# Attention scores from chunk 5 on as one float32r product a head, over q and k stacked three times

## The reference

```python
# q, k, v: (4, 8, 768, 40); i_gate, f_gate: (4, 8, 768); all float32
for t in range(S):
    m_new = np.maximum(f_gate[:, :, t] + m, i_gate[:, :, t])
    f_stab = np.exp(f_gate[:, :, t] + m - m_new)
    i_stab = np.exp(i_gate[:, :, t] - m_new)
    m = m_new
    C = f_stab[:, :, None, None] * C + i_stab[:, :, None, None] * np.einsum('bhd,bhe->bhde', vt, kt)
    n = f_stab[:, :, None] * n + i_stab[:, :, None] * kt
    h_tilde = np.einsum('bhde,bhe->bhd', C, qt)
    nq = np.einsum('bhd,bhd->bh', n, qt)[:, :, None]
    y[:, :, t] = sigmoid(o_gate[:, :, t]) * h_tilde / np.maximum(np.abs(nq), 1.0)
x = y as (3072 tokens, 320)
h = x @ w_in; g = np.maximum(h, 0) + alpha * np.minimum(h, 0)   # 320 -> 2048
x = g @ w_out                                                  # 2048 -> 320
h = np.maximum(np.maximum(x @ w1, x @ w2), x @ w3)             # 320 -> 768, three times
out = h @ w_out2                                               # 768 -> 320
```

## Time and profile before

| what | value |
|---|---|
| median of 3 runs | 748.95 us |
| profiled execution's own time | 748.46 us |
| its span (first to last instruction) | 746.7 us |
| PE busy | 737.6 us (99%) |
| PE weight loads busy | 652.4 us (87%) |
| DVE busy | 455.0 us (61%) |
| ACT busy | 306.9 us (41%) |
| POOL busy | 175.4 us (23%) |
| moved by DMA | 55.66 MB, mean 75 GB/s |

### The profile page before, as it was taken

One profiled execution on the slowest core, in us unless ns is written; L12 is line 12 of the kernel. 1 busy time (PEld: TensorE's weight loads), 2 busy tenths in 40 slices (PEclk: granted clock), 3 DMA queues, 4 the chain that ended last, 5 costly groups with the idle time before them and its releaser, 6 DMA issues.

```text
span 746.7 us, 11542 instructions
## 1 busy us (share of the span) xinstructions
PE 737.6 (99%) x4430; PEld 652.4 (87%) x4430; DVE 455.0 (61%) x774; ACT 306.9 (41%) x646; POOL 175.4 (23%) x201
## 2 busy tenths in 40 slices
PE   8899999999999999999999999999999999999998
PEld 6899999999988888888888888888888888888886
DVE  7787787799778868776877548633242424324232
ACT  6675744645564446444643446311212112121211
POOL 6697154164243324332431000000000000000000
PEclk9999999999999999999999999999999999999999
DMA  9973322423223213221200270030202002000101
GB/s 237 287 206 110 120 67 66 124 71 98 96 86 105 75 39 119 92 87 35 67 2 0 103 218 0 1 120 2 77 1 77 1 1 78 1 35 1 36 1 35
DMA packets 30407, 55.66 MB, mean 75 GB/s; under 512 B 3176, under 2 KB 19024, under 8 KB 29968
## 3 DMA queue, kind: packets, MB, share of 16 engines
q1 hardware_dynamic: 29888, 54.49, 23.8%
q10 hardware_dynamic: 464, 0.43, 0.2%
HBM read 46.96 MB, written 7.95 MB: 74 GB/s over the span
## 4 chain that ended last, share of the span: by engine, by line
PE 90%; DVE 4%; POOL 2%; issue 2%; ACT 2%; DMA 1%; SPq 0%; DVEq 0%; ACTq 0%; POOLq 0%
PE bank L794 26%; PE bank L757 22%; PE bank L680 6%; PE bank L772 6%; PE bank L774 5%; PE bank L773 5%; PE bank L809 3%; PE bank L810 3%; PE bank L811 3%; PE bank L776 3%; PE bank L777 3%; PE bank L688 2%; PE bank L696 1%; PE bank L718 1%; PE bank L730 1%
## 5 line engine op out<-in xcount | busy, mean ns | idle before, releaser
L757 PE MATMUL bank<-x_split,w_hi 128*128 128x512 f32 (+2 forms) x560 | 167.4, 366 | 2.0 <-ACT x_split L898 2.0
L757 PE MATMUL bank<-x_split,w_lo 128*128 128x512 f32 (+2 forms) x336 | 120.1, 360 | 0.0
L940 ACT ACTIVATE g_full<-bank 128x512 f32<-128x512 f32 (+2 forms) x112 | 59.8, 534 | 135.4 <-PE bank L757 134.4
L757 PEld LDWEIGHTS bank<-x_split,w_hi 128*128 128x128 f32 x560 | 102.6, 189 | 14.5 <-ACT x_split L898 2.2
L1184 DVE SCALAR_TENSOR_TENSOR g_full<-g_full,beta,bank 128x512 f32<-128x512 f32 (+2 forms) x112 | 74.6, 666 | 40.7 <-ACT g_full L940 40.1
L1165 DVE TENSOR_TENSOR g_lo<-g_full,g_hi 128x512 fp32r<-128x512 f32 (+2 forms) x112 | 79.5, 710 | 32.5 <-ACT g_hi L949 31.7
L1205 DVE TENSOR_TENSOR best<-bank,first_of_max 128x512 f32<-128x512 f32 x36 | 24.9, 692 | 102.5 <-PE bank L794 76.1
L772 PE MATMUL bank<-g_hi,wproj 128*128 128x512 f32 (+2 forms) x224 | 83.9, 374 | 0.8 <-DVE g_lo L1165 0.8
L949 ACT ACTIVATE g_hi<-g_full 128x512 fp32r<-128x512 f32 (+2 forms) x112 | 63.1, 564 | 48.1 <-DVE g_full L1184 47.9
L774 PE MATMUL bank<-g_hi,wproj 128*128 128x512 f32 (+2 forms) x224 | 80.5, 359 | 0.0
L773 PE MATMUL bank<-g_lo,wproj 128*128 128x512 f32 (+2 forms) x224 | 80.3, 358 | 0.0
(11 more groups left out here) (135 smaller groups left out, 1379.7 us busy)
## 6 DMA issues: line engine op xcount, KB each, us to landing
u_bcast<-u_scratch SPq DMA_DIRECT2D x21, 512.0 KB, 3.9
kv<-in_kv SPq DMA_DIRECT2D x24, 324.0 KB, 3.0
q_t<-in_q_t SPq DMA_DIRECT2D x24, 180.0 KB
k_t<-in_k_t SPq DMA_DIRECT2D x72, 60.0 KB
out<-final SPq DMA_DIRECT2D x5, 640.0 KB, 3.8
wproj_raw<-in_w_out SPq DMA_DIRECT2D x4, 640.0 KB, 11.1
o_gate<-in_o_gate SPq DMA_DIRECT2D x4, 640.0 KB, 4.5
w_raw<-in_w_max SPq DMA_DIRECT2D x2, 1152.0 KB, 6.4
```

The costliest lines, as they stand in the source:

```text
L757: ins = pe.matmul(ps[:, 0:cols], w[:, a, f], xs[:, x, 0:cols], start=(m == 0), stop=(m == 7))
L940: act.activation(gf[:, n % GF_SLOTS, 0:cols], hid[j % HID_BANKS][:, 0:cols], ACT.Relu, scale=-1.0).then_inc(neg_done, 1)
```

## The change

From chunk 5 (`STACK`) on, q and k come from HBM transposed, 40 rows for all 8 heads side by side, three times below each other (120 x 1024 values, 480 KB each), into one buffer `qk_raw` (it lies where the k slots were, so it is filled after the last plain scores). ACT copies both into float32r tiles `qk_terms`, with a sign by row: q as (high, high, -high), k as (high, -high, high). Then a masked add turns the negative rows into low parts: DVE does q (one scalar_tensor_tensor over 120 x 1024), POOL does k (a product with a row mask, then an add, over 120 x 1024 each). One float32r matmul a head over the 120 rows then gives high x high + high x low + low x high. The per-slot k loads go away for these chunks; q stays, for `carry`.

```diff
 def chunk_groups(ch):
...
-    return [[("scores", ch)] + soon * [("prepare", ch + 1)], [("carry", ch)],
+    stack, begin = STACK < ch + 1 < NCH, ch + 1 == STACK
+    return [[("scores", ch)] + soon * [("prepare", ch + 1)], [("carry", ch)] + stack * [("high", ch + 1)],
             [("values", ch)] + more * [("gate", ch + 1, 0)],
             more * [("gate", ch + 1, 1)] + [("finish", ch, 0)],
-            [("finish", ch, 1)] + pack * [("pack", ch + 1, 0)] + later * [("prepare", ch + 2)],
-            pack * [("pack", ch + 1, 1)]]
+            [("finish", ch, 1)] + begin * [("high", ch + 1)] + stack * [("low", ch + 1)]
+            + pack * [("pack", ch + 1, 0)] + later * [("prepare", ch + 2)],
+            begin * [("low", ch + 1)] + pack * [("pack", ch + 1, 1)]]
...
+        raw, kt_at = sb("qk_raw", [128, 2, H, L], F32)
+        terms3, _ = sb("qk_terms", [128, 2, H, L], F32R)
...
             eng.dma_start(qt[0:KR, c, :, :], q_t[ch]).then_inc(qk_loaded[c], 16)
-            for a in range(KH):
-                eng.dma_start(kt[a * D:(a + 1) * D, c, a * NK:(a + 1) * NK, :], k_t[ch, a]).then_inc(qk_loaded[c], 16)
+            if ch < STACK:
+                for a in range(KH):
+                    eng.dma_start(kt[a * D:(a + 1) * D, c, a * NK:(a + 1) * NK, :], k_t[ch, a]
+                                  ).then_inc(qk_loaded[c], 16)
...
+        def load_raw(eng, ch):
+            eng.wait_ge(scored, NG * STACK)
+            wait(eng, q_terms, ch - STACK)
+            wait(eng, k_terms, ch - STACK)
+            for n in range(2):
+                eng.dma_start(raw[0:KR, n, :, :].rearrange("p h t -> p (h t)"), qk[ch - STACK, n]
+                              ).then_inc(raw_loaded, 16)
...
                 load_chunk(sp, ch)
                 load_u(sp, ch)
+                if ch > STACK:
+                    load_raw(sp, ch - 1)
...
-                    pe.wait_ge(qk_loaded[c], QK_LOADS * nth)
+                    if ch < STACK:
+                        pe.wait_ge(qk_loaded[c], qk_loads(ch))
+                    else:
+                        pe.wait_ge(q_terms, ch - STACK + 1)
+                        pe.wait_ge(k_terms, ch - STACK + 1)
...
+                            if ch < STACK:
+                                lhs, rhs = kt[0:KR, c, h % KH * NK + h // KH, :], qt[0:KR, c, h // KH, :]
+                            else:
+                                lhs, rhs = terms3[0:KR, 1, h, :], terms3[0:KR, 0, h, :]
...
+                if kind == "high":
+                    act.wait_ge(raw_loaded, 32 * (n + 1))
+                    act.wait_ge(scored, NG * ch)
+                    act.activation(terms3[0:KR, 0, :, :], raw[0:KR, 0, :, :], ACT.Copy, scale=sign[0:KR, 1:2]
+                                   ).then_inc(qk_high, 1)
+                    act.activation(terms3[0:KR, 1, :, :], raw[0:KR, 1, :, :], ACT.Copy, scale=sign[0:KR, 0:1]
+                                   ).then_inc(qk_high, 1)
...
+                if kind == "low":
+                    dve.wait_ge(qk_high, 2 * (ch - STACK) + 1)
+                    dve.scalar_tensor_tensor(out=terms3[0:KR, 0, :, :], in0=raw[0:KR, 0, :, :], scalar=own[0:KR, 0, 2:3],
+                                             in1=terms3[0:KR, 0, :, :].bitcast(F32), op0=ALU.mult, op1=ALU.add
+                                             ).then_inc(q_terms, 1)
...
+                if kind == "low":
+                    pool.wait_ge(qk_high, 2 * (ch - STACK) + 2)
+                    link(pool.tensor_scalar(raw[0:KR, 1, :, :], raw[0:KR, 1, :, :], own[0:KR, 0, 1:2], None, ALU.mult))
+                    pool.tensor_tensor(terms3[0:KR, 1, :, :], raw[0:KR, 1, :, :], terms3[0:KR, 1, :, :].bitcast(F32),
+                                       ALU.add).then_inc(k_terms, 1)
```

More of the change, by code:

```diff
@@ L63 @@
 UNSPLIT = FIRST[2]
+STACK = UNSPLIT
+TERMS = 3
 STILL = 18
@@ L67 @@
 RING_BANKS = 3
-QK_LOADS = 16 * (1 + KH)
 CREDIT2 = 2
@@ L183, with qk_loads @@
 W2_LOW_AT = {5: (0,), 6: (1, 2), 7: (3, 4), 8: (5, 6), 9: (7, 8), 10: (9, 10), 11: (11,)}
+def qk_loads(ch):
+    return sum(16 * (1 + KH) if n < STACK else 16 for n in range(ch % SLOTS, ch + 1, SLOTS))
 class Links:
@@ L211, in of_heads, with build @@
     return ps.rearrange("p (g w) -> p g w", g=NK)[:, :, 0:KH * DE].rearrange("p g (k d) -> p g k d", k=KH)
-def build(nc, f_g, i_g, q_t, k_t, kv, o_g, w_in, w_out, alpha, w_max, w_out2, out):
+def build(nc, f_g, i_g, q_t, k_t, qk, kv, o_g, w_in, w_out, alpha, w_max, w_out2, out):
     with ExitStack() as ctx:
@@ L350, in build @@
         qk_loaded = [sem(f"qk_loaded{c}") for c in range(SLOTS)]
+        raw_loaded = sem("raw_loaded")
+        sign_set = sem("sign_set")
+        qk_high = sem("qk_high")
+        q_terms = sem("q_terms")
+        k_terms = sem("k_terms")
         u_loaded = [sem(f"u_loaded{c}") for c in range(SLOTS)]
@@ L535, in _ @@
                             load_o(sp, b + 3)
+            load_raw(sp, NCH - 1)
             sp.wait_ge(x_ready, NCH)
@@ L679, in attention @@
                             h = g * HG + k
-                            ins = pe.matmul(ps[:, k * L:(k + 1) * L], kt[0:KR, c, h % KH * NK + h // KH, :], qt[0:KR, c, h // KH, :],
-                                            start=True, stop=True)
+                            if ch < STACK:
+                                lhs, rhs = kt[0:KR, c, h % KH * NK + h // KH, :], qt[0:KR, c, h // KH, :]
+                            else:
+                                lhs, rhs = terms3[0:KR, 1, h, :], terms3[0:KR, 0, h, :]
+                            ins = pe.matmul(ps[:, k * L:(k + 1) * L], lhs, rhs, start=True, stop=True)
                         ins.then_inc(scored, 1)
@@ L877, in attention @@
                 nth = ch // SLOTS + 1
+                if kind == "high":
+                    n = ch - STACK
+                    if n == 0:
+                        act.wait_ge(sign_set, 1)
+                    act.wait_ge(raw_loaded, 32 * (n + 1))
[4 more added lines that the diff above has]
+                                   ).then_inc(qk_high, 1)
                 if kind == "sigmoid":
@@ L1063, in attention @@
                 kind = step[0]
-                if kind in ("prepare", "gate", "pack", "sigmoid", "exps", "turns", "bcast", "products"):
+                if kind in ("prepare", "high", "gate", "pack", "sigmoid", "exps", "turns", "bcast", "products"):
                     return
@@ L1101, in attention @@
                     dve.wait_ge(alpha_loaded, 16)
+                    dve.tensor_scalar(sign[:, :], own[:, 0, 1:3], -2.0, 1.0, ALU.mult, ALU.add).then_inc(sign_set, 1)
                     link(dve.tensor_scalar(beta[:, :], alpha_sb[:, :], -1.0, 1.0, ALU.mult, ALU.add))
@@ L1387, in nine, with three @@
         return rows.reshape(NCH, NK, KH, D, L)
+    def three(x):
+        rows = chunks(x).transpose(0, 2, 4, 1, 3).reshape(NCH, D, H * L)[STACK:]
+        return np.concatenate([rows] * TERMS, axis=1)
     arrays = {
@@ L1393 @@
         "q_t": nine(q).transpose(0, 2, 3, 1, 4).reshape(NCH, KR, NK, L),
-        "k_t": nine(k).transpose(0, 2, 3, 1, 4),
+        "k_t": nine(k).transpose(0, 2, 3, 1, 4)[:STACK],
+        "qk": np.stack([three(q), three(k)], axis=1),
         "kv": np.concatenate([tokens(k), tokens(np.concatenate([v, np.ones_like(v[..., :1])], axis=3))], axis=2),
```

5 lines of the change are left out of this document (4 added, 1 removed).

## The result

The changed kernel takes **838.98 us** (median, 837.87 to 839.89) against 748.25 for the kernel before, a ratio of 1.121 (95% interval 1.119 to 1.123). The forecast was 757 with a range of 742 to 770: the side was right, the size was not. The loss is 91 us instead of 8.

A forecast was written before the change was run, and what follows sets the result against it. PE, busy 99% of the span, was taken as the bound. The terms -16.2 + 14.6 + 5.2 + 2.1 + 2.5 + 1.6 gave +9.8 us, 758.8 on the median's scale, less 2 for overlap: 757 us, range 742 to 770.

The forecast's parts named there:

- The gain: Scores on PE: 8 float32r records of 106 ns replace 16 float32 ones, 0.85 us a chunk, 19 chunks, -16.2 us.
- both rivals on the width: Scores on PE: narrow float32r as slow as float32, 770 us, chance 0.14; or quicker weight load, 753 us, chance 0.08.
- (a): First chunk change in each block: q's low part comes late behind ACT's gapless run, lengthened by the copies; +14.6 us.
- (d): POOL against DVE: POOL's extra work slows DVE by 0.5 us in five of ten waiting chunks; +2.5 us, 0 to 8.
- (b): Later chunk changes in a block: PE's scores wait for q's low part behind `y`, or for the buffer loop; +5.2 us.
- (b), the loop: One buffer, low part to low part: 15 us; waits of 1.95 and 1.2 us in block 2, hidden in 512-column blocks.
- the loop binds everywhere: Rival: slower loads or locked-out DVE make the buffer loop cost 2 us more at 14 chunks; 775 us, chance 0.06.
- (c): End of block 0: the first copies on ACT have no cover; +2.1 us, 0 to 3.3.
- (e): PE's granted clock: one fall to half speed for 3.3 us after a wait; +1.6 us, 0 to 6.
- The rival on the clock: The clock falls at all five long waits instead of one, 4 x 1.6 us more; 763 us, chance 0.09.
- The far end of the gain: Scores on PE at 0.06 us a head: the gain's far end is -22 us, another 6 us on PE.
- What would show it: Signs in the later profile; forecast wrong if low-part waits sum below 14 us or POOL's low part of k comes last.

The follow-up runs named there:

- compute_q: The changed kernel without the loads after chunk 5's and without POOL's low part of k; copies and q's low part stay: 773.2 us.
- load_once: The changed kernel with q and k loaded once, for chunk 5; copies and low parts still made for every chunk: 800.3 us.
- warm_q: compute_q plus 72 float32r products of 512 columns, sums thrown away, put into PE's six long waits: 764.0 us (ratio 1.019 to 1.022).
- the versions with moves: Against the changed kernel: q and k loaded once in 80 rows, laid into 120 rows by six SBUF moves; 742.6 to 802.5 us by order and first chunk.

## Why the forecast missed

*The gain* (-16.2): 14.9 us in 18 chunks, 15.7 for 19. Right, and with it 0.106 us a record; both rivals on the width are out.

*(a), the first chunk change of a block* (+14.6): 15.7 us without POOL's work (`compute_q`), so the part with ACT's run was right. In the whole change it is 24.6, and the same without the loads (24.7, `load_once`): 9 us come from DVE's waits for POOL, which (a) left to (d).

*(b)*: the waits behind `y` read from the earlier trace rows are right in order and low in sum (7.3 us measured without the loop, 4.8 read). DVE's low part took up to 2.1 us beside POOL and not 1.2, which accounts for part of it.

*(b), the loop* is the step that failed first. The forecast made it 15 us and called it hidden in the blocks of 512 columns. It is 20.2: issue and loads 6.5 instead of 5.0 (the upper end, 6.2, was in the text, and not used), copies 2.2 instead of 2.1, and from the split to the end of the low part 11.6 instead of 8.0. Of these last 3.6 us 1.8 are `g_lo` at 2.40 instead of 0.60, 1.3 the two `norm` at 0.96 and 0.68 instead of 0.17. The rival "the loop binds everywhere" had the mechanism, at a chance of 0.06 and 2 us a chunk; inside a block it exceeds the old distance of the later chunks, 17 us and less, by 3 us and more. The working of that rival is off too: 2 us at 14 chunks are 28, and even less the 5.2 of (b) that makes 780, not 775.

*(c)* (+2.1): the copies cost 1.2 us there (`compute_q`, 82.02 against 80.80); the other 4.5 us of 5.7 came with POOL's work, as a stop of PE and a lower clock behind it.

*(d), POOL against DVE* (+2.5) failed as well, by two sizes. POOL needs 5.3 us a chunk, not 3.5 to 4.6, and a meeting costs up to 1.9 us (`g_lo`, `inner`), not 0.5; and it was counted in waiting chunks only, where it also lengthens the loop. The loads and POOL's work together are 65.8 us (`compute_q` to the whole change) against 3 forecast, 2.5 for POOL and 0.5 for the loop: 23.1 are waits for q's low part, 16.8 waits for `g_lo` in the stretch of the stacked chunks, 20.2 the clock, 4.5 the end of block 0, and 1.2 the rest. A sum of separate terms could not show the 28.6 us that only exist together.

*(e), the clock* (+1.6): 14.4 us without loads and POOL's work, 34.6 with them. One fall was taken, where six waits of 1.41 to 4.53 us in `compute_q`, straight out of dense work, were each followed by a lower clock. The rival on the clock was right in kind and is worth 9 us (`warm_q`), not 6; in the whole change it comes on top of waits that the forecast did not have.

*The far end of the gain*: 0.06 us a head would save another 0.046 x 152 = 7 us and not 6, so the end is -23. Nothing hangs on it.

*What would show it*: neither sign named for a wrong forecast came. The waits for the low parts were above 14 us, and POOL's low part was not the last, so these signs could not have shown this failure. Another did: ACT was to stand before its copies for the loads in block 2 only, and stood 13 times, in the later blocks too, 66.1 us in sum.

## What to carry to other kernels

A buffer that is filled again only when its last reader is done makes a loop; write it down whole (reader, issue, load, each engine's queue in between), with every piece at its upper end, and compare it with the period, before any wait is priced alone. Look for an engine that awaits the load with other work queued behind the wait: in the versions with moves a few steps in the order were worth 18 us. Work given to an idle GpSimd was paid here by VectorE, which waited for whole instructions, in the loop and outside it. Before a wait is put down to a loop, take one member out and look at each wait by its place: the longest one here, 7.1 us, stayed as it was when the loads were left out.
